# Retention, two MLPs on one core: loads sent two at a time, weights split a turn later

## What is computed

```python
scores = (1 / sqrt(64)) * q @ k.T            # batch 2, heads 8, sequence 576, head size 64
ret = scores * D                             # D[i, j] = gamma_h ** (i - j) for i >= j, else 0
x = (ret @ v)                                # to 1152 tokens x 512 features
out = sum_e p[:, e] * (relu(x @ w1[e]) @ w2[e])          # 4 experts, 512 -> 1024 -> 512
h = out @ w_in                               # 512 -> 2048
y = (h * tanh(softplus(h))) @ w_out          # 2048 -> 512
```

## Time and profile before

| | us |
|---|---|
| median of 3 runs | 621.29 (620.27 to 621.33) |
| the profiled execution | 619.39 |
| its span in the trace | 617.3 |
| PE busy | 604.9 (98%) |
| DVE, ACT, POOL busy | 265.1, 234.8, 278.5 |

### The profile page before, as it was taken

The page is one execution under the profiler, slowest core; times in us unless marked ns, Lnnn a source line. Parts: engine busy times, 40 slices in busy tenths (PEclk is TensorE's granted clock), DMA queues, the critical chain, the costliest instruction groups (busy, mean ns, idle before and its releaser), DMA issues.

```text
span 617.3 us, 9709 instructions
## 1 busy us (share of the span) xinstructions
PE 604.9 (98%) x3952; PEld 546.4 (89%) x3952; DVE 265.1 (43%) x365; ACT 234.8 (38%) x434; POOL 278.5 (45%) x230
## 2 busy tenths in 40 slices
PE   7799999999999999999999999999999999999997
PEld 5788999999899999999999999989989999989996
DVE  5477654323254433154434154535545432334334
ACT  2466244322233321323332223435455454334431
POOL 2668645534435535335554435532446543443300
PEclk9899999999999999999999999999999999999999
DMA  9963222322112332012331112321112232201002
GB/s 345 340 225 103 72 66 65 109 72 64 35 34 69 107 100 69 34 35 69 102 102 54 50 35 69 103 68 52 52 35 65 67 101 75 69 0 52 2 0 103
DMA packets 24923, 50.47 MB, mean 82 GB/s; under 512 B 2864, under 2 KB 2992, under 8 KB 24880
## 3 DMA queue, kind: packets, MB, share of 16 engines
q1 hardware_dynamic: 24736, 49.84, 25.2%
q10 hardware_dynamic: 144, 0.02, 0.0%
HBM read 47.49 MB, written 2.36 MB: 81 GB/s over the span
## 4 chain that ended last, share of the span: by engine, by line
PE 95%; DMA 2%; issue 1%; DVE 1%; SPq 1%; ACT 1%
PE bank L527 31%; PE bank L529 31%; PE bank L528 31%; DMA w_raw<-in_weights 2%; PE bank L651 1%; PE bank L459 1%; PE bank L489 1%; PE bank L493 1%; SPq L423 0%; DVE acc_sb L945 0%; DVE acc_sb L949 0%; PE bank L464 0%; SPq L420 0%; ACT st L728 0%; ACT xa_hi L734 0%
## 5 line engine op out<-in xcount | busy, mean ns | idle before, releaser
L412 POOL TENSOR_TENSOR w_lo<-w_raw,w_hi 128x512 fp32r<-128x512 f32 x96 | 134.4, 1414 | 147.8 <-ACT w_hi L385 144.3
L527 PE MATMUL bank<-w_hi,h_hi 128*128 128x512 f32 x432 | 168.7, 390 | 0.0
L529 PE MATMUL bank<-w_hi,h_lo 128*128 128x512 f32 x432 | 168.4, 390 | 0.0
L528 PE MATMUL bank<-w_lo,h_hi 128*128 128x512 f32 x432 | 168.3, 390 | 0.0
L932 DVE TENSOR_TENSOR h_act<-part,bank 128x384 f32<-128x384 f32 x96 | 52.9, 552 | 170.4 <-PE bank L529 169.9
L407 POOL TENSOR_TENSOR ws<-ws_f,ws 128x1024 fp32r<-128x1024 f32 x24 | 58.4, 2432 | 144.8 <-ACT ws L381 144.8
L529 PEld LDWEIGHTS bank<-w_hi,h_lo 128*128 128x128 f32 x432 | 81.1, 188 | 16.9
L528 PEld LDWEIGHTS bank<-w_lo,h_hi 128*128 128x128 f32 x432 | 81.1, 188 | 12.3
L527 PEld LDWEIGHTS bank<-w_hi,h_hi 128*128 128x128 f32 x432 | 81.0, 188 | 12.1
L764 ACT ACTIVATE part<-bank 128x384 f32<-128x384 f32 x72 | 35.4, 491 | 138.8 <-PE bank L529 138.8
L899 DVE SCALAR_TENSOR_TENSOR h_lo<-h_act,h_hi 128x384 fp32r<-128x384 f32 x64 | 73.3, 1155 | 20.9 <-ACT h_hi L754 20.3
(11 more groups left out here) (98 smaller groups left out, 867.6 us busy)
## 6 DMA issues: line engine op xcount, KB each, us to landing
w_raw<-in_weights SPq DMA_DIRECT2D x144, 256.0 KB, 2.7
loaded<-in_toks SPq DMA_DIRECT2D x9, 512.0 KB, 7.7
loaded<-in_feats SPq DMA_DIRECT2D x8, 512.0 KB, 7.0
out<-acc_sb SPq DMA_DIRECT2D x6, 256.0 KB, 2.1
out<-acc_sb SPq DMA_DIRECT2D x1, 768.0 KB, 3.5
loaded<-in_first SPq DMA_DIRECT2D x1, 726.0 KB, 4.5
ident<-in_ident SPq DMA_DIRECT2D x1, 64.0 KB, 4.7
p_nat<-in_probs ACTq DMA_DIRECT2D x1, 18.0 KB, 5.3
```

The costliest lines, as they stand in the source:

```text
L412: pool.tensor_tensor(w_lo[layer][:, x], w_raw[:, r % RAW], w_hi[layer][:, x].bitcast(F32), ALU.subtract).then_inc(s_wl, 1)
L527: pe.matmul(out, w[0], x[0], start=first, stop=False, **more)
L528: pe.matmul(out, w[0], x[1], start=False, stop=False, **more)
L529: return pe.matmul(out, w[1], x[0], start=False, stop=last, **more)
```

## The change

Line numbers in the order rows below are those of each file; `job_hi` and `job_lo` stand at the same lines in both.

- SP: one weight load goes out ahead of chunk 4, where two did. From then on every load waits until the last but one before it has landed: the features of chunk c wait for the tokens of chunk c-1, the tokens for a weight, the next weight for the features. The five turns carry five weight loads (1 to 5), the prologue load 0. Loads 6 to 13 are paced in the same way. The load of `ident` moves from after chunk 8 to behind load 13.
- The jobs of `w1` tiles 0 to 6 move one turn later (tile 7 stays in turn 6). The tiles `w2` 0 to 5 come a place later too: turn 7 has `w2` 0, `w2` 1 and the sum job, so `w2` 2 now comes behind the sum job.
- ACT: in turn 3 the first job goes ahead of the high part of tile 0.
- POOL: in each turn the jobs go ahead of `v_decay(c + 2)`.

```diff
--- before.py
+++ after.py
@@ -58,11 +58,11 @@
 
 TILE_AMID = {3: 0}
 TILES_IN = {3: (1,), 4: (2,), 5: (3,), 6: (4,), 7: (5, 6), 8: (7,)}
-JOBS_IN = {1: (("w1", 0, 0),), 2: (("w1", 0, 1), ("w1", 0, 2)), 3: (("w1", 0, 3),), 4: (("w1", 0, 4), ("w1", 0, 5)),
-           5: (("w1", 0, 6),), 6: (("w1", 0, 7), ("w2", 0, 0)), 7: (("w2", 0, 1), ("w2", 0, 2), ("s", 0, 0)),
-           8: (("w2", 0, 3), ("w2", 0, 4)), 9: (("w2", 0, 5),)}
-
-WEIGHTS_IN = (2, 2, 2, 2, 2)
+JOBS_IN = {2: (("w1", 0, 0),), 3: (("w1", 0, 1), ("w1", 0, 2)), 4: (("w1", 0, 3),), 5: (("w1", 0, 4), ("w1", 0, 5)),
+           6: (("w1", 0, 6), ("w1", 0, 7)), 7: (("w2", 0, 0), ("w2", 0, 1), ("s", 0, 0)),
+           8: (("w2", 0, 2), ("w2", 0, 3)), 9: (("w2", 0, 4), ("w2", 0, 5))}
+
+PACED = 14
 ROWS_IN = {4: 5, 5: 6, 6: 7, 7: 8}
 PROBS_IN = 5
 WARM_START, WARM_NEXT = 7, 5
@@ -429,21 +429,32 @@
                 sp.dma_start(w_raw[:, r % RAW], weights_in[2 * UNITS * e + UNITS * layer + u])\
                   .then_inc(s_raw[r % RAW], 16)
 
+            def weights_there(r):
+                sp.wait_ge(s_raw[r % RAW], 16 * (r // RAW + 1))
+
             sp.dma_start(loaded[:, lead - CONSTS:lead + 2 * KIND], first_in).then_inc(s_feats[0], 16)
             load_toks(0)
             for c in range(1, SLOTS):
                 load_feats(c)
                 load_toks(c)
-            at = 0
+            load_weights(0)
             for c in range(SLOTS, PLACES):
-                for r in range(at, at + WEIGHTS_IN[c - SLOTS]):
-                    load_weights(r)
-                at += WEIGHTS_IN[c - SLOTS]
+                at = c - SLOTS + 1
+                if c == SLOTS:
+                    sp.wait_ge(s_feats[(c - 1) % SLOTS], landed(c - 1))
+                else:
+                    sp.wait_ge(s_toks[(c - 1) % SLOTS], landed(c - 1))
                 sp.wait_ge(s_o, c - SLOTS + 1)
                 load_feats(c)
+                weights_there(at - 1)
                 load_toks(c)
-            sp.dma_start(ident[:, :], ident_in).then_inc(s_id, 16)
-            for r in range(at, len(LOADS)):
+                sp.wait_ge(s_feats[c % SLOTS], landed(c))
+                load_weights(at)
+            for r in range(PLACES - SLOTS + 1, len(LOADS)):
+                if r < PACED:
+                    weights_there(r - 2)
+                if r == PACED:
+                    sp.dma_start(ident[:, :], ident_in).then_inc(s_id, 16)
                 load_weights(r)
             by_rows = out.rearrange("(g p) d -> p g d", p=P)
             sp.wait_ge(s_af, read(EXPERTS - 1, TT - 1))
@@ -790,9 +801,12 @@
                 for job in IN_TURN.get(c - 1, ()):
                     if JOBS[job][0] == "s":
                         job_hi(act, job)
+                ahead = 1 if c in TILE_AMID else 0
+                for job in IN_TURN.get(c, ())[:ahead]:
+                    job_hi(act, job)
                 if c in TILE_AMID:
                     plain_hi(*divmod(TILE_AMID[c], ITEMS))
-                for job in IN_TURN.get(c, ()):
+                for job in IN_TURN.get(c, ())[ahead:]:
                     if JOBS[job][0] != "s":
                         job_hi(act, job)
             for n in range(4):
@@ -1098,10 +1112,10 @@
             v_decay(0)
             v_decay(1)
             for c in range(TURNS):
+                for job in IN_TURN.get(c, ()):
+                    job_lo(pool, job)
                 if c + 2 < PLACES:
                     v_decay(c + 2)
-                for job in IN_TURN.get(c, ()):
-                    job_lo(pool, job)
             pool.wait_ge(s_tl, 4)
             for s in range(1, ALL_STAGES):
                 for job in IN_STAGE.get(s, ()):
```

## The result

The changed kernel takes 629.6 us (median of 5 runs, 628.3 to 630.61). The kernel before, run beside it, takes 621.04 us (5 runs, 619.92 to 621.33). The ratio is 1.014, with a 95% interval of 1.0122 to 1.0158. So the change costs 8.6 us, where I forecast 1.2, and 629.6 lies outside my range of 619.0 to 624.8. The profiled execution took 628.3 us with a span of 626.2, 8.9 more than before.

A forecast was written before the change was run, and what follows sets the result against it. PE, busy 98% of the span, bounds the kernel. A 5.8 us early gain is nearly all spent by turn 7 waiting behind weight 5; `w2` 2 starts 1.2 us late: 621.29 + 1.2 = 622.5 us, range 619.0 to 624.8.

The forecast's parts named there:

- PE's stall near 18.9 us: PE's longest issue wait, 2.33 us from 18.85 us; forecast to fall under 1 us with the clock at 1.0.
- Rival 3: Slower by much: weight 5 lands at 41.6, adding 1.4 us, plus a clock fall; 623.3 to 625.0 us, chance 0.25.
- the price of a landing: Issue to landing with two loads in flight: 3.5 us for 512 KB, 2.6 for 256 KB, putting weight 5 at 40.2.
- the floors and wake-ups in my working: Each load lands no sooner than the last plus its transfer (1.3 or 0.65 us); SP's wake-up costs 0.05 us.
- an upper bound for 512 KB: Landing price of 512 KB: at most 3.7 us, the fastest features load seen; lower bound 3.3.
- From the landing of weight 5 to `state_copy(7)`: ACT and DVE work behind weight 5's landing at 40.2, which puts `state_copy(7)` at 46.4, against 45.91 before.
- DVE's part: DVE's work from tile 3's low part to `decayed(6)`: 3.55 us, ending at 45.6.
- 57.74 + 1.3 to 1.8: `w2` 2's low part, now behind the sum job on POOL: done at 59.05 to 59.55 us, before turn 7's +0.5.
- PE has no wait at `w2` 2: Sign in the profile that the forecast is wrong towards faster; forecast there was a wait of about 1.2 us.
- 5.8 us of gain on PE up to tile 7: PE earlier by 5.8 us at tile 7 if issue waits from 18.85 us on went and the clock stayed up.
- an extra 1.7 us for a fall of the clock: PE's clock falling after its wait of 3 us and more ahead of `scores_and_state(7)`: costs 1.7 us, 1.4 to spare.
- My reading: PE's issue waits, 4.8 us in all, are waits for its next instructions, whose load waits behind data on the DMA queue.

The follow-up runs named there:

- Run 6: The changed kernel with one load in flight, each load waiting for the one right before it; 653.57 us (one run).
- Run 9: Loads only, no computation: 24 loads each with one, two and three in flight; a turn of three loads takes 9.5, 5.92 and 4.8 us.
- run 7: The changed kernel with 24 matmuls of zeros on PE ahead of `scores_and_state(7)`; 629.46 us, ratio 1.0153.
- run 12: The changed kernel (two loads in flight) with weight 5's job moved from turn 5 to turn 6; 628.41 us, ratio 1.0132.
- run 3: The changed kernel's new job tables and orders with the old loads: two weights a chunk, no waits on landings; 620.89 us, ratio 1.0.
- run 2: The changed kernel with three loads in flight, each load waiting for the last but two; 621.17 us, ratio 1.0004.
- run 5: The changed kernel with three loads in flight and `w2` 2 split ahead of the sum job; 620.97 us, ratio 1.0007.
- run 11: The changed kernel with three loads in flight, `w2` 2 ahead of the sum job and weight 5's job in turn 6; 619.99 us, ratio 1.0001.
- run 4: The kernel before with only the pace added: each load waits for the last but one, two weights a turn, old tables; 627.64 us, ratio 1.0104.
- run 8: The changed kernel with the small load of the probabilities (`p_nat`) issued in turn 1 instead of turn 5; 629.43 us, ratio 1.0147.
- run 13: No computation of the reference: 40 loads of 512 KB without waits beside 2500 matmuls; PE stood still seven times, 0.86 to 1.23 us each, while the queue was full.
- run 10: Loads only, with one, two and three in flight, beside 5000 short matmuls on PE; a turn of three loads takes 10.2, 6.0 and 5.3 us.
- run 1: The changed kernel without its waits for landings, one weight a turn and new tables kept; 623.11 us, ratio 1.003.

## Why the prediction was wrong

**The place and the mechanism were right.** PE's stall near 18.9 us went and the clock stayed at 1.00 there. Two in flight set a pace, the pace set weight 5, ACT stood still until it landed (5.95 us), `scores_and_state(7)` waited for `v_decay(7)`, and the loss reached the second layer, where PE and the low part of `w2` 2 came within 0.1 us of each other. Rival 3 named it as the slower side, from too small a landing (41.6 us for weight 5).

**The term that failed is the price of a landing.** I wrote: "For 256 KB I take 2.6 us", and for 512 KB "I take the middle, 3.5". In the chain the three weights took 3.62, 3.46 and 3.49 us and the five chunk loads 4.02, 4.70, 4.47, 5.65 and 3.50. Together they took 32.9 us, where my prices in the same chain make 5 x 3.5 + 3 x 2.6 = 25.3. That is 7.6 more; the floors and wake-ups in my working had covered 1.9 of it, and 5.7 are left: 45.97 against 40.2. Run 6 shows that 3.5 and 2.6 are prices of a load alone. I had a term for a second load only as a floor ("the landing of the last plus its own transfer"), and took the later of the two. Run 9 shows that both slow down together: its prices, put into the same working, give weight 5 at 45.0.

**So both ends of the range were wrong as well.** I called 3.7 us an upper bound for 512 KB, because it was the fastest of eight in a deep queue. A fastest landing bounds a price from above only for a load that is no more crowded than that one. With 4.3, 4.4 and 2.9 us, the medians of run 9, a turn takes 5.9.

**Two smaller terms.** From the landing of weight 5 to `state_copy(7)` I had 6.2 us and it took 7.0. DVE's part was 4.6 us and not 3.55: `row_decay` took 1.23 us (0.89 before) and `p_norm` 0.98 (0.20 before). For `w2` 2, "57.74 + 1.3 to 1.8", with turn 7 at +7.3 and 1.85, gives 66.9; the rule was right. The wait there was not 1.2 us but 0.1, as PE came late itself; the sign "PE has no wait at `w2` 2" therefore did not tell faster from slower.

The sum with the measured numbers: weight 5 5.8 us later than predicted, then 0.8, makes `state_copy(7)` 6.6 later than my 46.4, at 53.0. Of the 1.2 us forecast for `w2` 2 and these 6.6, plus 0.3 for the low part (1.85, where I had 1.55) and 0.2 more for the sum job, come 8.3, which makes 66.9 of my 58.6; PE started it at 67.03. (In the timeline the kernel before has 58.42 and not 58.6, so the distance is 8.6.)

**What was gained upstream did not help.** I reckoned 5.8 us of gain on PE up to tile 7, and 3 to 4 of them spent in the wait for weight 5. With weight 5 5.8 us later that wait should have been about 9 us; it was 5.4. PE had lost some of its lead earlier: it waited 1.52 us for the low part of a tile at 35.33 us, and ran at half clock from 35.9 to 39.3. What was left it could not use.

**The clock.** I gave rival 3 an extra 1.7 us for a fall of the clock after the wait. The clock fell, and for longer (46.1 to 56.4 us), but run 7 shows that it lay beside POOL's work and cost nothing of its own that can be measured. That is no rule for this kernel: in run 12 the fall comes behind the wait for `w2` 2, with nothing beside it, and its eight slow matmuls take 3.3 us where full speed takes 1.8.

**The waits on "issue".** My reading holds in the main. PE has 4.8 us of them before, 5.6 without a pace and 4.4 in run 3; with three in flight 4.4, 2.4 and 1.7 (runs 2, 5 and 11); with two 1.7 in the changed kernel and 2.3, 3.3, 2.7 and 0.5 in runs 4, 7, 8 and 12. So they grow with the loads in flight, but one profile is no measure of them; run 13 turns them on and off. Even so, no kernel that keeps the loads early and has fewer of these waits (run 11) is measurably faster. In run 11 PE waits 2.3 us for a low part of a weight and 1.3 for one of the inputs, which the kernel before does not have: its gain is taken by the waits that come next.

**Open.** Of the 6.5 us a turn, 0.5 are explained by no run. They are no accident of one profile: by the same two issues of features, runs 7, 8 and 12 have 6.6, 6.7 and 6.4, with weight 5 at 47.2, 47.2 and 45.9. Single landings also move between kernels whose loads wait on the same landings: the tokens of chunk 7 took 5.65 us in the changed kernel and 4.85 in run 12 (issued at 33.72, the features of chunk 8 behind them at 38.57).

## What to carry to other kernels

A wait that holds loads to a number in flight lets the landing time set the pace of the program: reckon the turn from landings measured at that same number in flight, and expect them to be longer than those of a load alone. If such a price isn't in the trace, its upper end can lie well above the shortest landing seen (3.7 us here; with two in flight a landing of 512 KB took up to 5.65). Before throttling a queue to free an engine from stalls, find the first wait behind it that the later data will reach, since what the engine gains is lost there.

## What the runs showed of the hardware

- Three loads of 512, 512 and 256 KB take 9.5 us with one in flight, 5.92 with two and 4.8 with three. The second saves 3.6 us, the third 1.1; the moved rates are 138, 222 and 273 GB/s, against 397 to 407 with a deep queue.
- PE's waits on "issue" stand 256 instructions apart behind a deep queue of data, 0.86 us or more each, and are gone when the queue is empty (run 13). With two or three loads in flight and the same matmuls (run 10) PE was busy for 48.19 of 48.19 and 42.55 of 42.66 us.
- A small DVE operation took five times as long when one of POOL's was under way at its start. `p_norm`, 36 elements wide, ran from 49.83 to 50.81 in the changed kernel, and POOL's first low part from 49.47 to about 50.73. Before, POOL's next low part began only at 42.53, and DVE's timeline had:

```profile
42.32 0.20 DVE L986 TENSOR_TENSOR p_norm<-p_nat,p_inv 128x36 f32<-128x36 f32 x1
```

No run was made for this, but the traces of all twelve kernels that compute agree. In seven (the changed kernel and runs 1, 2, 5, 6, 7 and 8) a low part on POOL had begun 0.4 us before `p_norm`, and `p_norm` took 0.96 to 1.00 us and ended about when that low part did. In the other five no POOL operation was running when it began, and it took 0.20.
